# Fused local and coarse attention, expert layer and gated layer: heads of a pair change places in every second block of queries, and the lead's sums move to VectorE

## The reference

```
attention: coarse: q, k, v averaged over groups of 4 positions, full softmax(q k^T / 8) v,
                   each of the 144 results repeated 4 times
           local:  softmax over the keys with |i - j| < 4, times v
           out = coarse + local, as (4, 576, 512)
stage B:   x + relu(layernorm(x) * g @ w_ch1) @ w_ch2          w_ch1 512x2048, w_ch2 2048x512
stage C:   xk, xr = mixes of x with the position before it
           sigmoid(xr @ w_r) * (relu(xk @ w_k)^2 @ w_v)         w_k 512x1024, w_v 1024x512
```

## Time and profile before

| | |
|---|---|
| median of 3 runs | 808.15 us |
| the profiled execution | 809.56 us |
| its span, from the first to the last instruction | 807.8 us |
| TensorE busy | 786.5 us, 97% of the span |
| VectorE busy | 421.4 us, 52% |
| ScalarE busy | 274.5 us, 34% |
| POOL busy | 237.3 us, 29% |
| lead, up to the first matmul of L938 | 42.2 us |

### The profile page before, as it was taken

One profiled execution on the slowest core, in us unless ns is written; L12 is line 12 of the kernel. 1 busy time (PEld: TensorE's weight loads), 2 busy tenths in 40 slices (PEclk: granted clock), 3 DMA queues, 4 the chain that ended last, 5 costly groups with the idle time before them and its releaser, 6 DMA issues.

```text
span 807.8 us, 15879 instructions
## 1 busy us (share of the span) xinstructions
PE 786.5 (97%) x6492; PEld 717.0 (89%) x6492; DVE 421.4 (52%) x748; ACT 274.5 (34%) x655; POOL 237.3 (29%) x280
## 2 busy tenths in 40 slices
PE   5899999999999999999999999999999999999998
PEld 4689999999999999999999999997888888888886
DVE  3668654244544343553433423376577576675654
ACT  4465333133223223222222312355344333433322
POOL 6456753132434213334313213003111111111111
PEclk9999999999999999999999999999999999999999
DMA  9981350121450121152010000732003002010010
GB/s 192 242 249 29 76 99 24 35 43 33 70 99 31 23 44 45 31 96 58 2 37 30 2 13 10 279 107 80 3 0 105 1 0 80 1 52 1 1 53 26
DMA packets 115913, 48.50 MB, mean 60 GB/s; under 512 B 95616, under 2 KB 104832, under 8 KB 115840
## 3 DMA queue, kind: packets, MB, share of 16 engines
q1 hardware_dynamic: 115840, 47.49, 23.5%
HBM read 38.03 MB, written 9.44 MB: 59 GB/s over the span
## 4 chain that ended last, share of the span: by engine, by line
PE 94%; POOL 2%; DVE 1%; DMA 1%; ACT 1%; issue 1%; SPq 1%; POOLq 0%
PE psY L955 27%; PE psH L938 26%; PE psY L1008 12%; PE psH L989 12%; PE psA L971 6%; PE psA L871 3%; PE psA L844 2%; PE psA L796 1%; PE psA L823 1%; PE psA L855 1%; PE psA L809 1%; DMA v_first<-in_v_dram 1%; PE psA L881 1%; SPq L490 1%; DVE mixin L1478 1%
## 5 line engine op out<-in xcount | busy, mean ns | idle before, releaser
L1534 DVE SCALAR_TENSOR_TENSOR h_lo<-psH,h_hi 128x288 fp32r<-128x288 f32 x128 | 58.1, 454 | 230.7 <-ACT h_hi L1265 230.7
L955 PE MATMUL psY<-h_hi,w_hi 128*128 128x288 f32 x512 | 160.2, 313 | 0.0
L938 PE MATMUL psH<-xc_hi,w_hi 128*128 128x288 f32 x512 | 155.9, 304 | 2.4 <-DVE xc_lo L1416 2.4
L938 PE MATMUL psH<-xc_lo,w_hi 128*128 128x288 f32 x512 | 152.0, 297 | 0.0
L938 PE MATMUL psH<-xc_hi,w_lo 128*128 128x288 f32 x512 | 151.6, 296 | 0.0
L955 PE MATMUL psY<-h_lo,w_hi 128*128 128x288 f32 x512 | 150.8, 294 | 0.0
L955 PE MATMUL psY<-h_hi,w_lo 128*128 128x288 f32 x512 | 150.7, 294 | 0.0
L1265 ACT ACTIVATE h_hi<-psH 128x288 fp32r<-128x288 f32 x128 | 52.5, 410 | 245.4 <-PE psH L938 245.4
L768 POOL TENSOR_TENSOR relu_k<-relu_k 128x512 f32<-128x512 f32 (+1 forms) x40 | 38.6, 966 | 255.8 <-ACT relu_k L1229 255.8
L955 PEld LDWEIGHTS psY<-h_hi,w_hi 128*128 128x128 f32 x512 | 96.2, 188 | 5.5 <-issue 2.7
L938 PEld LDWEIGHTS psH<-xc_hi,w_hi 128*128 128x128 f32 x512 | 97.2, 190 | 4.0 <-issue 2.6
(11 more groups left out here) (173 smaller groups left out, 1400.3 us busy)
## 6 DMA issues: line engine op xcount, KB each, us to landing
w_raw<-in_moe_w_ch_dram SPq DMA_DIRECT2D x8, 1024.0 KB, 7.0
v_win<-in_v_dram SPq DMA_DIRECT2D x84, 56.0 KB
x_scratch<-x SPq DMA_DIRECT2D x8, 576.0 KB, 3.6
out_dram<-gate SPq DMA_DIRECT2D x18, 256.0 KB, 2.2
raw<-in_q_dram SPq DMA_DIRECT2D x112, 36.0 KB, 2.6
raw<-in_k_dram SPq DMA_DIRECT2D x96, 36.0 KB, 1.9
v_raw<-in_v_dram SPq DMA_DIRECT2D x12, 288.0 KB
x_sh<-x_scratch SPq DMA_DIRECT2D x3, 1026.0 KB, 5.7
```

Source lines behind the costliest of these rows:

```text
L938: ins = mm(psH[:, m % 2, 0:N], ws[a][:, kt, f * P:(f + 1) * P], xx[bb][:, kt], start=(kt == 0 and i == 0), stop=(kt == KT - 1 and i == 2))
L955: ins = mm(psY[:, d, 0:N], ws[a][:, f, d * P:(d + 1) * P], hs[bb][:, m % 2], start=(f == 0 and i == 0), stop=(f == NF1 - 1 and i == 2))
L1534: nc.vector.scalar_tensor_tensor(out=h_lo[:, m % 2], in0=psH[:, m % 2, 0:N], scalar=0.0, in1=h_hi[:, m % 2].bitcast(F32), op0=ALU.max, op1 ...
```

## The change

1. The output bank of scores is `par ^ bl` in place of `par`. So in block 1 the heads of a pair have changed places, in the probabilities and, after the transpose, in the partitions of the keys.
2. v's windows are loaded to rows 64 * (par ^ bl), and values read keys and v there. The output partitions stay at 64 * par; block bl now goes to bank bl. `x_o` therefore reads two banks, with one addition for each block.
3. All five sums of the lead run on VectorE as `tensor_reduce`; POOL's `sum_first` and its semaphore go. The sums of x for unit 0 run on VectorE too (`x_sum_first`).
4. In the lead's lists, ScalarE takes the first coarse exponentials before the copy of the first transposed probabilities, VectorE takes `sum_of_p(0, 1)` between the two `top_of_d`, and the splits of w1's first part stand between the values' steps.

```diff
@@ load_window
-                        sp.dma_start(vw_slot(w)[RB * par:RB * par + KB, b],
+                        row = RB * (par ^ b)
+                        sp.dma_start(vw_slot(w)[row:row + KB, b],
@@ POOL: sum_first is taken out; its list
             v_sum(0, 0)
-            sum_first("Tk", 1)
-            sum_first("Tq", 1)
             v_sum(0, 1)
-            sum_first("Tk", 2)
             norm(0, 0)
             v_sum(0, 2)
             norm(0, 1)
             v_sum(0, 3)
-            for n in range(NW_U):
-                x_sum(0, n)
@@ scores_d
-                if u == 0:
-                    pe.wait_ge(pool_summed, POOL_SUMS)
-                pe.wait_ge(summed, DVE_SUMS + (flipped_by(u) if u else 0))
+                pe.wait_ge(summed, N_TURN0 + (flipped_by(u) if u else 0))
@@ scores
-                            ins = mm(pairs[pair_at(i)][RB * bl:RB * bl + nq, par, j * KB:(j + 1) * KB], qT[rows, j, q0:q0 + nq],
+                            ins = mm(pairs[pair_at(i)][RB * bl:RB * bl + nq, par ^ bl, j * KB:(j + 1) * KB], qT[rows, j, q0:q0 + nq],
@@ values
-                        keys = slice(RB * par, RB * par + KB)
                         for bl in range(BLOCKS):
+                            row = RB * (par ^ bl)
+                            keys = slice(row, row + KB)
                             at = j * ROWS + bl * RB
-                            ins = mm(pairs[pair_at(i)][D * par:D * par + D, 0, j * W + bl * BQ:j * W + (bl + 1) * BQ],
+                            ins = mm(pairs[pair_at(i)][D * par:D * par + D, bl, j * BQ:(j + 1) * BQ],
                                      vw_slot(w)[keys, bl, j, :], pt[keys, at:at + BQ], start=True, stop=True, skip_group_check=True)
@@ ScalarE's list
             exp_first(1)
+            exp_d(0, 0)
             pt_o(0, 0)
-            exp_d(0, 0)
             exp_d(0, 1)
             exp_first(2)
             pt_o(0, 1)
+            hi_weight("w1", 0, 0)
             od_o(0, 0)
             od_o(0, 1)
-            hi_weight("w1", 0, 0)
+            hi_weight("w1", 0, 1)
             pt_o(0, 2)
-            for kt in range(1, KT):
-                hi_weight("w1", 0, kt)
+            hi_weight("w1", 0, 2)
+            hi_weight("w1", 0, 3)
@@ x_o
-                src = pairs[pair_at(i)][:, 0, 0:KT * W].rearrange("p (j g t) -> p j g t", j=KT, t=FACTOR)
-                up = odT[:, :, n * GW:(n + 1) * GW].unsqueeze(3).to_broadcast([P, KT, GW, FACTOR])
-                dst = x[:, u % 2, :, n * W:(n + 1) * W].rearrange("p j (g t) -> p j g t", t=FACTOR)
-                nc.vector.tensor_tensor(dst, src, up, ALU.add).then_inc(x_made, 1)
+                for bl in range(BLOCKS):
+                    src = pairs[pair_at(i)][:, bl, 0:KT * BQ].rearrange("p (j g t) -> p j g t", j=KT, t=FACTOR)
+                    t0, ng = n * W + bl * BQ, BQ // FACTOR
+                    up = odT[:, :, t0 // FACTOR:t0 // FACTOR + ng].unsqueeze(3).to_broadcast([P, KT, ng, FACTOR])
+                    dst = x[:, u % 2, :, t0:t0 + BQ].rearrange("p j (g t) -> p j g t", t=FACTOR)
+                    ins = nc.vector.tensor_tensor(dst, src, up, ALU.add)
+                ins.then_inc(x_made, 1)
+
+            def x_sum_first(n):
+                dve.wait_ge(x_made, n + 1)
+                if n == 0:
+                    dve.wait_ge(consts, 6)
+                at = slice(n * W, (n + 1) * W)
+                chain(nc.vector.tensor_tensor(xs[:, :, at], x[:, 0, 0:2, at], x[:, 0, 2:4, at], ALU.add))
+                nc.vector.tensor_tensor(xs[:, 0, at], xs[:, 0, at], xs[:, 1, at], ALU.add).then_inc(x_summed, 1)
@@ VectorE's list
             mask(0, 0)
+            sum_first("Tk", 1)
+            sum_first("Tq", 1)
             mask(0, 1)
             sum_of_p(0, 0)
             mask(0, 2)
+            sum_first("Tk", 2)
             top_of_d(0, 0)
+            sum_of_p(0, 1)
             top_of_d(0, 1)
-            sum_of_p(0, 1)
@@ VectorE's list, the end of the lead
             norm_first(2)
+            lo_weight("w1", 0, 0)
             x_o(0, 0)
+            x_sum_first(0)
             x_o(0, 1)
-            lo_weight("w1", 0, 0)
+            x_sum_first(1)
+            lo_weight("w1", 0, 1)
             x_o(0, 2)
-            for kt in range(1, KT):
-                lo_weight("w1", 0, kt)
+            x_sum_first(2)
+            lo_weight("w1", 0, 2)
+            lo_weight("w1", 0, 3)
```

More of the change, by code:

```diff
@@ L93, in fused_kernel @@
     N_TURN0 = len(turns)
-    DVE_SUMS, POOL_SUMS = 2, N_TURN0 - 2
     SQ = 32
@@ L275, in fused_kernel @@
         turned = sem("turned")
-        pool_summed = sem("pool_summed")
         turn_out = sem("turn_out")
@@ L658, in v_sum @@
                                         ALU.add).then_inc(vd_made, 1)
[L660 to L672, removed]
             def norm_d(u, n):
@@ L694, in x_sum @@
                 pool.wait_ge(x_made, w + 1)
-                if w == 0:
-                    pool.wait_ge(pool_summed, POOL_SUMS)
                 if u >= 1 and n == 0:
```

## The result

| | before | after |
|---|---|---|
| median, first measurement | 809.01 us (4 runs) | 795.81 us (4 runs, 793.75 to 796.80) |
| ratio, 95% interval | | 0.9833 (0.9803 to 0.9863) |
| ratio in a second measurement (e12) | | 0.9829 (0.9808 to 0.9849) |
| profiled execution (span) | 809.56 (807.8) us | 796.80 (794.7) us |
| TensorE busy | 786.5 us | 774.3 us |

The time fell by 1.7%, 12.8 us between the two profiled executions, where 15.3 had been forecast (792.9 us, range 788.5 to 798.5). The four steps of the forecast that matter can be read one by one. The changed kernel's lines are shifted: scores are L821, values L849, transposes of probabilities L832, coarse scores L773, `up_b` L916, `down_b` L933, VectorE's maximum L1355, `x_o` L1382.

The account below looks back on a forecast made before the run. TensorE's own stream, 94% of the chain, was taken as the bound. Values -11.1, x_o +0.3 and the lead -4.5 gave -15.3 us: from the median 808.15 to 792.9 us, range 788.5 to 798.5.

Parts of the forecast that it names:

- values, 21 windows: TensorE's values steps after the lead fall from 1.10 to 0.57 us on four quarters, saving 11.1 us.
- late transposes: Halved x_o ends 0.11 us later, so transposes wait at a few tight places; 0.3 us given back in all.
- lead, up to the first up_b: Everything before the main loop's first matmul gets 4.5 us shorter, through steps a to d.
- rival A: Quarters share by rows alone: values stay at 1.10 us, time 806.5 us; chance 0.07.
- rival B: Two row groups writing one bank hold each other apart: scores 1.22 us, values gain nothing, time 821; chance 0.03.
- the line of 0.8 ns a column: Values, scores and coarse values: time per record on a part of the array grows 0.8 ns a column, from 69 ns at 48.
- The bound taken from the scores' row: Values step after the change: bound of 0.61 us, from scores, whose columns are more; 0.57 was taken.
- step a: Lead, sums moved to VectorE: scores_d starts at about 18.0 and not 19.24, 1.25 us earlier.
- Steps b and c: Lead: exponentials before the copy, values 0 at 22.3; then TensorE's row with shorter values, no prob_first wait, ends at 32.3.
- Step d: End of the lead: x_o, VectorE's sums and the last two lo_weight, then centring at 35.3 and not 39.76.
- Clock: Stretch at the lower level from 562.4 us costs about 1.7 us and may come or stay away; 1.7 either way.

Follow-up runs that it names:

- e12: The changed kernel itself measured once more, on the same chip as e11: ratio to before 0.9829, 795.14 us.
- e9: Changed kernel with values' 16 calls in three other orders, one for each window of units 1 to 7: steps of 0.61, 0.66 and 1.41 us.
- e6: Changed kernel with values' calls reordered, all of block 0 before block 1, so two quarters in turn: 0.88 us a step, ratio to before 0.9909.
- e11: Changed kernel with x_o as one addition over both banks and POOL's second and third part of v delayed: ratio to before 0.9834, 795.97 us.
- e4: Changed kernel with values streaming 48, 64 and 32 columns in the three windows of units 1 to 7: steps of 0.61, 0.62 and 0.60 us.
- e10: Kernel before, values in units 1 to 7 with block outside head, as before, and with 32 columns: 1.07, 1.10 and 1.07 us a step.
- e2: Only the exchange of places and the halved x_o, with the lead of the kernel before: ratio to before 0.9857, values 0.61 us.
- e1: Only the lead's lists and sums, with operands, banks and x_o of the kernel before: ratio to before 0.9966, values 1.10 us.
- e5: Changed kernel with POOL's v_sum(0, 1) behind norm(0, 0) and VectorE's third maximum: main loop 32.5 us behind the first transpose.
- e8: Changed kernel with VectorE's centring and split of x ahead of the last two lo_weight: one execution took 798.86 us.

## Why the prediction came out as it did

The sum, term by term, in us, measured in the one pair of profiled executions:

| term | forecast | measured |
|---|---|---|
| values, 21 windows | -11.1 | -10.3 (0.49 each, not 0.53) |
| late transposes | +0.3 | +0.34 (0.26, 0.04, 0.04) |
| lead, up to the first up_b | -4.5 | -3.6 |
| slow form of the first main matmuls | not in the sum | +0.3 |
| together | -15.3 | -13.2 (span -13.1, executions -12.8) |

**Right:** that the quarters carry the gain and that rival A (rows alone) and rival B (banks) do not hold; scores did not move (0.61), and runs of either order of rows and columns are the same in e9. The Trainium skill's rule in "TensorE: Matmul & The Clock Gate", section "Part 3: Packing small matmuls — row/col tiling", that a weight load overlaps only across row groups, does not decide here. Scores and the changed values change row group every 4 records, as values before did, and take 0.61 against 1.10; e6, whose row group changes every 2, takes 0.88. The forecast's own argument against rival B, that values and coarse values lie on one line per record, was worth little, since that line was chance; the rival falls by the scores. What the Trainium skill says in "TensorEngine Tiling (Array Packing)", section "Gotcha 1: PSUM Pressure", of row tiles that cannot access one bank at the same time does not show as a cost where the partitions differ: scores write one bank from two row groups after the change and keep their 0.61.

**The place of the three late transposes** was read from their slack and came as worked out: one of 0.26 in unit 1, two of 0.04 where a transpose of raw stands before `x_o`. Their cause is only in part the halved addition: with one addition (e11) 0.20 of the 0.26 are left. That much is the earlier transpose meeting a VectorE that POOL holds up; the same TENSOR_SCALAR took 1.29 us before the change too (81.68), where there was room for it.

**Off in size, values:** the line of 0.8 ns a column through 48, 56 and 72 columns led to 8 x 69 = 0.55. e4 and e10 show that columns count neither on four quarters (0.60 to 0.62 for 32 to 64) nor, to speak of, on two (1.07 and 1.10 for 32 and 48). The line was chance; the bound taken from the scores' row was the value, and the forecast of 0.57 lay between the two. That costs 0.04 x 21 = 0.8 us.

**Off in size, the lead:** step a left a cost out. It took VectorE's queue as the sum of its rows and put nothing down for POOL's additions beside it. The trace of before had it to be read, a TENSOR_SCALAR of 0.50 us that ends at 15.24 and a POOL addition that ends at 15.22:

```profile
14.74 0.50 DVE L1376 TENSOR_SCALAR top<-top 112x8 f32<-112x8 f32 x1
```

```profile
14.39 0.83 POOL L671 TENSOR_TENSOR xs<-qT 128x384 f32<-128x384 f32 x1
```

So coarse scores came at 19.17 and not at 18.0. Steps b and c fitted: values 0 came 4.29 us behind the coarse scores (4.3 forecast), the mean 10.05 behind values 0 (10.0). Step d came 0.3 better: centring 2.7 us behind the last values step, 3.0 forecast. The first transpose came 0.4 us later in this execution, and step a lost 0.8 beyond that; less step d's 0.3 this is the missing 0.9. Most of that 0.9 is this one execution. Told from the first transpose the forecast put the coarse scores at 13.3 us and the main loop at 33.0; the four profiles with this lead have 13.4 to 14.1 and 32.8 to 33.5, 33.1 in the mean, where the two with the lead of before (before and e10) have 37.5 and 37.3. That is a gain of 4.3 us, near the 4.5 of the forecast. Part of it is luck: step a's missing cost, 0.1 to 0.8 us from execution to execution, is made up for by a step d that was put too dear.

**Clock:** before and after, 3.4 us near the start of stage C run at the lower level. The rows of the changed kernel and of e2, same stretch, with the granted clock behind the engines' busy times:

```profile
545.00:556.00 11.00, 9.17 (x33) 6.99 (x32) 9.62 (x18) 7.91 (x14) 2.47 (x2) 0.84 0.42 146
```

```profile
545.00:556.00 11.00, 9.17 (x40) 7.10 (x39) 10.22 (x20) 8.71 (x15) 2.47 (x2) 1.00 0.44 149
```

In 11 us TensorE began 33 matmuls in the one and 40 in the other, at seven times about 0.23 us some 1.6 us. The same wait of 1.8 us stands in front of the stretch in both. It comes in six of the 14 profiles (before, the changed kernel, e1, e5, e6, e12) and not in the others, whichever kernel it is, so it is a part of the spread of 3 us between runs, and no part of the change.

## What to carry to other kernels

Small products on quarters of the array: count how many different quarters a few successive records stand on; going from two to four took 1.10 us to 0.61, while columns from 32 to 64 and a second output bank made no difference. Interleave them closely: the same four quarters in runs of 8 took 1.41. Before work is moved to VectorE, look at what POOL runs beside it, and before a POOL instruction is delayed, at which VectorE instruction it will meet next.

## What the runs showed of the hardware that was not expected

- On two quarters, 16 records of 64 weight columns on each, a step takes 1.07 to 1.10 us for 32 as for 48 streamed columns: 67 to 69 ns for each record of a quarter. On four quarters 32 records never went below 0.60 us, 19 ns each.
- The order of the same 16 calls on four quarters counts: 0.61, 0.66, 0.88 and 1.41 us in four orders. It reads as if work on another quarter overlaps only a few records ahead.
- VectorE's TENSOR_SCALAR on SBUF did not end before POOL's TENSOR_TENSOR beside it: in all 14 profiles, between 13 and 26 us, each one that took over 0.3 us (42 of them) ended 0.02 to 0.03 us after one of POOL's. It took up to 1.55 us (e6) in place of 0.17. TENSOR_REDUCE kept its length.
- Two waits of 0.49 and 0.73 us in the first matmuls of the main loop went with 13.6 us in the slow form, in one execution (e8), where the others had 2.9 to 6.0.
